# Sign bits in the second score product of a bucketed attention, ahead of two dense layers

## What is computed

```python
q_bits = (np.einsum('bhsd,dk->bhsk', q, proj) > 0).astype(np.int64)
k_bits = (np.einsum('bhsd,dk->bhsk', k, proj) > 0).astype(np.int64)
q_bucket = np.sum(q_bits * powers, axis=-1)
k_bucket = np.sum(k_bits * powers, axis=-1)
mask = q_bucket[:, :, :, None] == k_bucket[:, :, None, :]
scores = scale * np.matmul(q, k.transpose(0, 1, 3, 2))
scores = np.where(mask, scores, -1000000000.0)
attn = np.exp(scores - np.max(scores, axis=-1, keepdims=True))
attn = attn / (np.sum(attn, axis=-1, keepdims=True) + 1e-09)
attn_out = np.matmul(attn, v)
```

## Time and profile before

| | us |
|---|---|
| median of three runs | 784.45 |
| the profiled execution | 782.37 |
| its span on the core | 780.6 |
| attention, to the first output matmul of the dense layers | 262.88 |
| from there to the end | 517.7 |
| TensorE busy (98% of the span) | 763.5 |
| DVE busy (52%) | 405.1 |
| ACT busy (44%) | 343.6 |
| POOL busy (37%) | 288.9 |

### The profile page before, as it was taken

The page is one execution under the profiler, slowest core; times in us unless marked ns, Lnnn a source line. Parts: engine busy times, 40 slices in busy tenths (PEclk is TensorE's granted clock), DMA queues, the critical chain, the costliest instruction groups (busy, mean ns, idle before and its releaser), DMA issues.

```text
span 780.6 us, 12163 instructions
## 1 busy us (share of the span) xinstructions
PE 763.5 (98%) x3800; PEld 644.7 (83%) x3800; DVE 405.1 (52%) x688; ACT 343.6 (44%) x657; POOL 288.9 (37%) x230
## 2 busy tenths in 40 slices
PE   7999999999999999999999999999999999999998
PEld 6788888888889888888888888888888888888886
DVE  5888887888898574343333432352323333242333
ACT  7988898888987221232212322132221312222121
POOL 3688878878897493000000366660000000000000
PEclk9999999999999999999999999999999999999999
DMA  6576667666762342000000032310001000010001
GB/s 168 136 148 167 146 141 177 151 127 157 157 120 61 84 136 82 1 0 1 1 0 1 27 100 89 107 55 0 1 1 42 11 0 0 0 54 0 0 0 54
DMA packets 46312, 52.77 MB, mean 68 GB/s; under 512 B 8912, under 2 KB 34768, under 8 KB 46288
## 3 DMA queue, kind: packets, MB, share of 16 engines
q1 hardware_dynamic: 46064, 52.13, 27.0%
q10 hardware_dynamic: 224, 0.33, 0.2%
HBM read 32.73 MB, written 3.19 MB: 46 GB/s over the span
## 4 chain that ended last, share of the span: by engine, by line
PE 75%; DMA 8%; POOL 6%; issue 5%; SPq 3%; DVE 2%; ACT 0%; POOLq 0%; DVEq 0%
PE acc L594 33%; PE h_ps L576 32%; DMA inv_dram<-row_inv 4%; DMA all_inv<-inv_dram 3%; PE pt_ps L542 2%; POOL wa_lo L431 2%; POOL kt L385 2%; PE pv_ps L556 2%; PE pv_ps L557 1%; PE s_ps L528 1%; PE s_ps L529 1%; POOL wa_hi L429 1%; POOL pt_hi L395 1%; DMA w_raw<-w_out_dram 1%; DVE w_raw L837 1%
## 5 line engine op out<-in xcount | busy, mean ns | idle before, releaser
L770 ACT ACTIVATE r_sb<-h_ps 128x512 f32<-128x512 f32 x96 | 57.4, 598 | 368.0 <-PE h_ps L576 368.0
L909 DVE TENSOR_SCALAR g_sb<-e_sb,sb_scale 128x512 f32<-128x512 f32 x48 | 27.9, 582 | 158.2 <-ACT e_sb L773 158.2
L907 DVE SCALAR_TENSOR_TENSOR g_sb<-e_sb,h_ps 128x512 f32<-128x512 f32 x48 | 33.0, 687 | 135.6 <-ACT e_sb L773 135.1
L804 DVE TENSOR_REDUCE row_min<-s_ps 128x1 f32<-128x768 f32 x96 | 91.5, 954 | 10.3 <-PE s_ps L529 9.6
L693 ACT ACTIVATE probs<-s_ps,row_min 128x768 f32<-128x768 f32 x96 | 87.0, 906 | 11.3 <-DVE row_min L804 9.3
L542 PE MATMUL pt_ps<-cst,probs 128*128 128x128 f32 x576 | 80.8, 275 | 0.7 <-DVE pt_lo L811 0.5
L556 PE MATMUL pv_ps<-pt_hi,v_nat 128*128 128x384 f32 x192 | 72.6, 378 | 7.8 <-DVE w_raw L837 7.7
L576 PE MATMUL h_ps<-xt_hi,wa_lo 128*128 (+1 forms) x192 | 74.7, 389 | 0.0
L576 PE MATMUL h_ps<-xt_lo,wa_hi 128*128 (+1 forms) x192 | 74.7, 389 | 0.0
L576 PE MATMUL h_ps<-xt_hi,wa_hi 128*128 (+1 forms) x192 | 74.7, 389 | 0.0
L576 PE MATMUL h_ps<-xt_hi,wb_hi 128*128 (+1 forms) x192 | 74.7, 389 | 0.0
(11 more groups left out here) (93 smaller groups left out, 1598.3 us busy)
## 6 DMA issues: line engine op xcount, KB each, us to landing
qt<-kt SPq DMA_DIRECT2D x45, 192.0 KB, 3.0
w_raw<-w_in_dram SPq DMA_DIRECT2D x32, 256.0 KB, 2.7
w_raw<-w_out_dram SPq DMA_DIRECT2D x32, 256.0 KB, 2.9
all_inv<-inv_dram SPq DMA_DIRECT2D x32, 192.0 KB, 3.7
raw<-qk_dram SPq DMA_DIRECT2D x15, 384.0 KB, 4.3
raw_v<-v_dram SPq DMA_DIRECT2D x16, 192.0 KB, 4.7
out_dram<-o_sb SPq DMA_DIRECT2D x12, 256.0 KB, 2.1
kt<-kt SPq DMA_DIRECT2D x15, 192.0 KB, 3.7
```

Source lines behind the costliest of these rows:

```text
L804: nc.vector.tensor_reduce(row_min[:, k:k + 1], s_ps[k % 2][:, :, 0:HALF], AX.XY, ALU.min).then_inc(min_done, 1)
```

## The change

**Bits in place of buckets.** Each head's six sign matmuls now stand together in the last unit of the head before (SIGN_UNIT). They make 108 rows in prep_ps: for either half of the tokens 12 rows for q and 12 for k, a bit and its opposite. One DVE operation writes them as 0 or 2^31 (for k -2^31) in fp32r (to_bits, write_bits). Four DMAs of 12 x 384 lay them in rows 64 to 75 of qt2 and kt2 (copy_bits), so the second score product, now over 76 rows, adds -2^62 for each bit in which q and k differ. Counts, onehots, penalties and the scaling of q are gone.

**Scores copied.** DVE multiplies the scores by -1/8 under a ceiling of 2^56, writes them to one of three buffers probs in SBUF and takes their minimum in the same operation (keep_scores); the exponential works in place there, and the next scores wait for the copy.

**Inverse.** POOL adds the epsilon (add_eps), and DVE takes the reciprocal in the first unit of the next group. The put writes single numbers to (t p) order, so that the normalise reads all_inv in sequence.

**Lists.** SyncE's pair and POOL's pair are ordered anew. Weights are loaded and split only in pairs 0 and 7, so five slots are loaded and four split when the attention ends (AMID = 4). In the first head the signs are two fp32 matmuls on the raw q and k (first_signs), and ACT, POOL and DVE make its parts; DVE, POOL, ACT and SyncE lists at the start follow that. WARM is 10 for 12.

SyncE's functions and its pair:

```diff
-            def copy_q(head, par):
-
-                hi, lo = kt1[par][low, :].bitcast(F32), kt2[par][low, :].bitcast(F32)
+            def copy_q_hi(head, par):
+
+                hi = kt1[par][low, :].bitcast(F32)
                 sp.wait_ge(qk_hi, head)
                 sp.dma_start(qt1[par][top, :].bitcast(F32), hi).then_inc(q_copied, 16)
                 sp.dma_start(qt2[par][top, :].bitcast(F32), hi).then_inc(q_copied, 16)
+
+            def copy_q_lo(head, par):
                 sp.wait_ge(qk_split, head)
-                sp.dma_start(qt1[par][low, :].bitcast(F32), lo).then_inc(q_copied, 16)
+                sp.dma_start(qt1[par][low, :].bitcast(F32), kt2[par][low, :].bitcast(F32)).then_inc(q_copied, 16)
...
-                sp.wait_ge(z_done, head + 1)
+                sp.wait_ge(z_done, head)
...
+
+            def copy_bits(head, par):
+
+                sp.wait_ge(bits_done, head)
+                for n in range(2):
+                    cols = slice(n * HALF, (n + 1) * HALF)
+                    for at, dst in ((n * HALF_ROWS, qt2), (n * HALF_ROWS + K_ROWS, kt2)):
+                        sp.dma_start(dst[par][bit_rows, cols].bitcast(F32),
+                                     bits[at:at + BIT_PAIR, :].bitcast(F32)).then_inc(bits_copied, 16)
...
-                sp.dma_start(inv_d[par].rearrange("(p t) -> p t", p=P),
-                             row_inv[:, (g % GROUPS) * HT:(g % GROUPS + 1) * HT]).then_inc(inv_out[par], 16)
+                sp.dma_start(inv_d[par].rearrange("(t p o) -> p t o", p=P, o=1),
+                             row_inv[:, (g % GROUPS) * HT:(g % GROUPS + 1) * HT].unsqueeze(2),
+                             allow_slow_non_contiguous=True).then_inc(inv_out[par], 16)
...
-            def pair(i, prev=True, nxt=True, after=True):
+            def pair(i, prev=True, nxt=True, after=True, weights=()):
                 copy_k(2 * i + 1, 1)
+                copy_bits(2 * i + 1, 1)
                 if prev:
+                    get_inv(i, -1)
                     move_second(i - 1, 0)
-                    get_inv(i, -1)
                 put_inv(i, 0)
                 load_v(2 * i + 1)
+                if weights:
+                    load_w(0, weights[0], 0, weights[0])
+                get_inv(i, 0)
                 if nxt:
-                    copy_q(2 * i + 2, 0)
+                    copy_q_hi(2 * i + 2, 0)
                 if prev:
                     move_second(i - 1, 1)
-                get_inv(i, 0)
+                if nxt:
+                    copy_q_lo(2 * i + 2, 0)
                 if after:
                     load_qk(2 * i + 4, 0)
-                if nxt:
-                    load_w(0, i + 1, 0, i + 1)
                 put_inv(i, 1)
                 if nxt:
                     copy_k(2 * i + 2, 0)
+                    copy_bits(2 * i + 2, 0)
+                get_inv(i, 1)
                 move_first(i, 0)
-                get_inv(i, 1)
                 put_inv(i, 2)
+                get_inv(i, 2)
                 if nxt:
                     load_v(2 * i + 2)
-                    copy_q(2 * i + 3, 1)
+                    copy_q_hi(2 * i + 3, 1)
                 move_first(i, 1)
-                get_inv(i, 2)
+                if nxt:
+                    copy_q_lo(2 * i + 3, 1)
                 if after:
                     load_qk(2 * i + 5, 1)
+                if weights:
+                    load_w(0, weights[1], 0, weights[1])
                 put_inv(i, 3)
```

POOL:

```diff
+            def add_eps(i, g):
+
+                c = slice(g * HT, (g + 1) * HT)
+                pool.wait_ge(exp_done, HT * (GROUPS * i + g) + HT)
+                pool.nop(nofuse=True)
+                nc.gpsimd.tensor_scalar(row_inv[:, c], row_sum[:, c], EPS, 1.0, ALU.add, ALU.mult).then_inc(sum_done, 1)
...
-            def pair(i, prev=True, nxt=True):
+            def pair(i, prev=True, nxt=True, weights=()):
                 split_third(i, 0)
-                split_w(at(wa_hi, i), at(wa_lo, i), i, 0, i + 1)
+                add_eps(i, 0)
+                if weights:
+                    split_w(at(wa_hi, weights[0]), at(wa_lo, weights[0]), weights[0], 0, weights[0] + 1)
+                if prev:
+                    split_x(i - 1, 0)
                 if nxt:
                     split_qk(2 * i + 2, 0)
+                add_eps(i, 1)
                 split_third(i, 1)
                 if prev:
-                    split_x(i - 1, 0)
+                    split_x(i - 1, 1)
                 split_third(i, 2)
+                add_eps(i, 2)
                 split_v(2 * i + 1, 1)
-                if prev:
-                    split_x(i - 1, 1)
+                if weights:
+                    split_w(at(wa_hi, weights[1]), at(wa_lo, weights[1]), weights[1], 0, weights[1] + 1)
                 if nxt:
                     split_qk(2 * i + 3, 1)
+                add_eps(i, 3)
                 split_third(i, 3)
                 if nxt:
                     split_v(2 * i + 2, 0)
...
-            pair(0, prev=False)
+            pair(0, prev=False, weights=(0, 1))
...
-            pair(PAIRS - 1, nxt=False)
+            pair(PAIRS - 1, nxt=False, weights=(2, 3))
```

TensorE:

```diff
+            def first_signs():
+
+                pe.wait_ge(planes_built, 4)
+                pe.wait_ge(k0_in, 16)
+                pe.wait_ge(q0_in, 16)
+                for n in range(2):
+                    last = mm(s_ps[1][0:K_ROWS + BIT_PAIR, n, 0:HALF], planes[:, 0:K_ROWS + BIT_PAIR],
+                              raw[0][:, n * HALF:(n + 1) * HALF], start=True, stop=True)
+                last.then_inc(z0_done, 1)
...
+                wait(pe, bits_done, head - 1)
                 dst = prep_ps[0:SIGN_ROWS, 0:HALF]
-                mm(dst, planes_hi[:, plane], kt1[par][:, cols], start=n == 0, stop=False)
-                mm(dst, planes_lo[:, plane], kt1[par][:, cols], start=False, stop=False)
-                if first:
-                    pe.wait_ge(lo0_done, n + 1)
-                last = mm(dst, planes_hi[:, plane], kt2[par][:, cols], start=False, stop=n == 1)
-                if n == 1:
-                    last.then_inc(z_done, 1)
...
-                mm(bank[:, 0:HALF], code[rows, :], bits[rows, :], start=True, stop=True).then_inc(counts_done, 1)
...
-                wait(pe, exp_done, u - 1)
+                wait(pe, scores_kept, u - 1)
                 q1 = qt1[par][:, t * P:(t + 1) * P]
-                q2 = qt2[par][:, t * P:(t + 1) * P]
+                q2 = qt2[par][score_rows, t * P:(t + 1) * P]
...
                     mm(s_ps[buf][:, n, 0:HALF], q1, kt1[par][:, cols], start=True, stop=False)
-                    last = mm(s_ps[buf][:, n, 0:HALF], q2, kt2[par][:, cols], start=False, stop=True)
+                    last = mm(s_ps[buf][:, n, 0:HALF], q2, kt2[par][score_rows, cols], start=False, stop=True)
...
-                        buckets_out(2 * head + 2)
                         pe.wait_ge(q_copied, 48 * head)
                         pe.wait_ge(k_copied, 16 * head)
+                        pe.wait_ge(bits_copied, 64 * head)
...
                 transpose_probs(i, u, k, 0)
                 transpose_probs(i, u, k, 1)
-                if follows and t == CODE_A:
-                    counts(head, 0)
-                if follows and t == CODE_B:
-                    buckets_out(2 * head + 1)
...
-                if follows and t == SIGN_B:
-                    if first and k == 0:
-                        signs(head, par, 0)
-                    signs(head, par, 1)
-                if more and t == SIGN_A:
-                    buckets_out(2 * head + 2)
-                    signs(head + 1, 1 - par, 0)
-
+                if first and k == 0:
+                    signs(head, par)
+                if more and t == SIGN_UNIT:
+                    signs(head + 1, 1 - par)
```

ACT and DVE:

```diff
-                act.wait_ge(min_done, u + 1)
-                wait(act, pt_done, 2 * u - 2)
-                nc.scalar.activation(probs[k % 2][:].rearrange("p (n c) -> p n c", n=2), s_ps[k % 2][:, :, 0:HALF],
-                                     ACT.Exp, bias=row_min[:, k:k + 1], scale=-1.0,
-                                     accum_out=row_sum[:, k, 0:1]).then_inc(exp_done, 1)
+                act.wait_ge(scores_kept, u + 1)
+                scores = probs[k % SRING]
+                nc.scalar.activation(scores[:], scores[:], ACT.Exp, bias=row_min[:, k:k + 1], scale=-1.0,
+                                     accum_out=row_sum[:, k:k + 1]).then_inc(exp_done, 1)
...
+            def to_bits(dst, z, rows):
+                return ts(dst, z, planes_in_sb[rows, C_THR:C_THR + 1], planes_in_sb[rows, C_AMP:C_AMP + 1], ALU.is_gt,
+                          ALU.mult)
+
...
             def write_bits(head):
...
+                rows = slice(0, SIGN_ROWS)
+                dve.wait_ge(z_done, head)
+                wait(dve, bits_copied, 64 * head - 64)
+                to_bits(bits[:], prep_ps[rows, 0:HALF], rows).then_inc(bits_done, 1)
+
+            def keep_scores(u, k):
+
```

(24 more changed lines are left out.)

318 lines of the change are left out of this document (146 added, 172 removed).

## The result

The changed kernel takes 978.56 us (median of four runs, 975.99 to 981.5), the kernel before 783.97 beside it: 1.248 times the time, 95% interval 1.244 to 1.252. The forecast was 775.0 with a range of 760 to 784. The profiled run has a span of 975.6 us.

A forecast was written before the change was run, and what follows sets the result against it. TensorE was taken to bound the attention, SyncE's queue second. Head -1.7, pair 0 -1.8, six pairs -10.6, last pair -0.4 and tail +5.0 made -9.5 from 784.45: 775.0 us, range 760 to 784.

The forecast's parts named there:

- The put: Inverse row sums to DRAM: 384 pieces of 4 bytes land in 4.3 us, bounds 3.8 and 6.2, for 3.8 before.
- The rival with the slow put: Inverse's way to DRAM: a put longer by x costs 13x; at 100 ns a piece 789.3 us; chance 0.15.
- TensorE bounds the attention, so work taken off it comes off the time: Attention: TensorE is the bound, SyncE's queue second; count matmuls, 0.45 us each, leave the path, 1.8 us per pair.
- the largest term, 10.6 us less in the six pairs: Six middle pairs: 28.7 us each against 30.46, 1.76 x 6 = 10.6 us less.
- SyncE's list in a middle pair: Middle pair: bits ready at 2.5 us, four bit DMAs to 4.7, then get and moves of x, landed at 9.05.
- New stall 1.4 us: Middle pair, unit 5: next head's signs wait 1.4 us for POOL's split of q and k, bounds 0.7 and 1.8.
- Head and pair 0: Start: 1.7 us less from shorter prologue and earlier score bank release, bounds 0 and 3; pair 0 loses its counts, 1.8.
- The tail: Before the first output matmul: last put waits for a weight split and lands behind 512 KB; 5.0 us more, bounds 1 and 7.
- DVE's copy of scores at 1.0 us: DVE in the attention: the copy with minimum takes 1.0 us, bounds 0.95 and 1.15, hidden under TensorE, booked at nothing.
- Signs with 108 columns and scores with 76 rows: TensorE in the attention: 108 columns for 44 and 76 rows for 128 cost nothing, matmuls staying 0.17 us apart.
- The weights not yet split: Dense layers: four slots ready for eight, splits hidden; uncovered up to 3.6 us per slot.
- the fourth rival: Tail: TensorE idles nearly 5 us, its clock halves; 2.7 us more per twelve matmuls, 777.7 us; 3 in 10 within the forecast.

The follow-up runs named there:

- e1: Changed kernel with the put back to 128 pieces of 12 bytes and the normalise reading with a stride; 819.44 us, 1.045 of the kernel before.
- e14: Changed kernel with the 12-byte put, SyncE's pair in the old order and two bit DMAs per head for four; 789.22 us, 1.0065 of the kernel before.
- e17: e15 with the sum and the reciprocal back on DVE in the last unit of a group; 788.32 us, 1.0073 of the kernel before.
- e15: e14 with the last pair's second weight split behind POOL's last sum and third, its load behind SyncE's moves; 786.5 us, 1.0031 of the kernel before.
- e2: Kernel before with only the put in 384 pieces of 4 bytes and the normalise reading in sequence; 916.59 us, 1.170 of the kernel before.

## Why the prediction was wrong

**The put: priced by the wrong time.** "I take 3.8 + 0.5 = 4.3 us, with bounds of 3.8 and 6.2" is the step that failed first: it measured 9.7. The 32 ns per piece of the earlier trace rows are the time that packets occupy a DMA engine; what SyncE waits for is the landing, and the row that held it, 3.8 us for 128 pieces, was not read as a price that depends on how the pieces lie. The trace of before has small neighbouring pieces in this one form only, and the bound was set by what a queue carries, not by what a write waits for. The rival with the slow put had the right side and the right place, at a chance of 0.15 and a price of 789 us. Its formula also fell: 13 x (9.7 - 4.3) = 70 us more would have been 845. It counted two delays per pair. In the new order all four puts of a pair follow each other in one list, and e1 to after is 19.5 us per pair (53.8 - 34.3), near to four times 6.1, less what is hidden.

**TensorE bounds the attention, so work taken off it comes off the time: wrong.** This is the deeper error, and the largest term, 10.6 us less in the six pairs, rests on it. They took 182.75 us with the counts, and 182.34 in e14, without counts and with the put of before. The stretches of the six pairs, before and in e14 (us, busy time and count of PE, PEld, DVE, ACT, POOL, then clock, DMA share, GB/s):

```profile
42.53:225.28 182.75, 175.51 (x1106) 155.34 (x1104) 153.64 (x277) 161.28 (x337) 151.47 (x132) 1.00 0.68 150
47.97:230.31 182.34, 168.36 (x1082) 159.94 (x1081) 145.74 (x312) 137.69 (x301) 135.28 (x142) 0.99 0.62 137
```

TensorE is busy for 7.1 us less and idle for 6.7 us more; its waits for normalised outputs in the pairs grew from 6.5 to 13.6 us. So the work that was saved came back as waiting. I read TensorE's busy time as the bound and booked nothing for what it would wait for next. What sets these waits in e14 is not settled. SyncE waits there for its own DMAs only 5.3 us, less than the 16.0 before, so it is not the list as in the kernel after. On the way to the normalised output POOL's sum and a reciprocal one unit later now stand ahead of the put and the get; e17 took both back, and 14.4 us of these waits stayed. No run takes the counts alone out of the kernel before.

**SyncE's list in a middle pair: wrong.** My walk had the bits ready at 2.5 and let four bit DMAs follow at once. The copy of k stands ahead of them, and it waits for copies of q that themselves now stand behind a get and its put. In e1 the first score matmul of a pair goes at 151.98 and the first bit DMA at 157.62: 5.6 us after it, not 2.5. "New stall 1.4 us" at the signs, behind POOL's split, did not come: TensorE was late by then. In its place there were 4.2 us of waits per pair in unit 4 (1.7 for the bits and 2.5 for the normalised output; 13.5 and 17.8 us in 8 and 7 waits in all) and half a clock behind them.

**Head and pair 0: wrong in sign.** The first scores start at 11.24 us (before: 10.34), the third ones at 14.16 for 13.35, still behind DVE for 1.36 us. Up to there 0.8 us were lost where I took 1.7 off. Pair 0 was to save 1.8 more. In e14 start and pair 0 take 47.97 us for 42.53, 5.4 more, which is the largest part of what e14 loses; TensorE's longest wait there, 3.2 us, is for an output of a group whose put stands behind 512 KB of weights. In e17 the stage takes 41.95, so the later reciprocal has a part in it.

**The tail: half right.** The last put behind a weight load that waits for a split is worth 2.7 us (e15 against e14, with the reservation made there) where I took 5.0, within the bounds of 1 and 7. In the kernel after the wait before the first output matmul is 6.3 us, with the slow put in it.

**Right:** DVE's copy of scores at 1.0 us. It takes 0.955 us with a row of its own of 0.083 for the accumulator, on DVE for the kernel after:

```profile
L813 DVE TENSOR_SCALAR_CACHE_REDUCE probs<-s_ps 128x768 f32<-128x768 f32 x96 | 91.6, 955 | 49.8 <-PE s_ps L562 48.6
...
L813 DVE DVE_READ_ACCUMULATOR probs<-s_ps 128x1 f32 x96 | 8.0, 83 | 0.0
```

The Trainium skill, "VectorE: DVE Perf Modes", section "Two Vector instructions with no wait between them", has it as two instructions; the trace agrees, at 83 ns and not ACT's 201. Together that is 1.04 us. TensorE hardly waited for DVE's splits, until e17 gave DVE more to do. Signs with 108 columns and scores with 76 rows cost nothing, at 0.17 us apart. The weights not yet split stayed hidden: the dense layers took 520.4 us for 517.7, and TensorE waited there for no split. The 2.7 us more are the fourth rival, the clock, at its price of 2.7 us for twelve matmuls: the first twelve, behind the wait of 6.3 us, start 0.43 us apart, not 0.23.

**The clock** was a rival for the tail alone. It came in every pair: the mean granted clock of each of e1's six middle pairs is 0.90, and in one of them, behind two waits, TensorE was granted 0.50 (1.2 GHz) for 4.3 us, and 1.00 again after it (us, busy time and count of five engines, clock):

```profile
160.00:166.20 6.20, 2.01 (x13) 1.43 (x11) 0.92 (x4) 2.86 (x6) 0.66 (x1) 0.84 0.52 85
166.20:170.50 4.30, 4.26 (x15) 4.20 (x16) 2.83 (x7) 1.57 (x4) 3.62 (x4) 0.50 0.72 151
```

Before that TensorE had been idle for two thirds of 6.2 us. 4.3 us at half clock are 2.15 us lost in this pair, an estimate from its row. Over the six pairs TensorE is busy for 179.5 us in e1 and for 168.4 in e14, 1.8 us a pair. So a stall that opens costs more than its own length.

## What to carry to other kernels

Price a small DMA write by its landing, not by the time its packets take, and measure it before it goes on a path that four waits per loop depend on; of the forms tried here, 4-byte pieces side by side in DRAM were the worst. Where one engine issues DMAs in order, read what it waits for: here it was other engines for most of the time before, and its own DMAs for 182 of 186 us of waits when its list held everything up; a get right behind its put then stops all else. Before work taken off the busiest engine is booked as gain, ask what that engine would wait for next: here 7.1 us of saved work became 6.7 us of waiting.

## What the runs showed of the hardware

- 384 pieces of 4 bytes side by side in DRAM land in 9.7 us, 64 bytes apart in 2.6, 512 bytes apart in 2.7; 128 pieces of 12 bytes side by side in 3.6. In the put looked at, the DMA engines are idle for 5.6 of 7.7 us.
- Other DMAs land later as well while such puts are under way: the copies of q took 5.9 us in the kernel after, 4.7 in e1; in the kernel before they took 3.0, and 7.9 with the put alone changed (e2). The Trainium skill, "DMA: Bandwidth & Descriptors", section "Queues, rings and completion order", has a semaphore's write wait for every earlier write of its DMA engine, which would give this; the runs don't show it apart from fuller queues.
- Score matmuls with 64 rows in turn with 128 start 0.37 us apart, with 76 rows 0.17. With 64 rows the load of the weights (0.18 to 0.19 us) starts together with its matmul's record, with 76 rows 0.17 us ahead of it. Why is not shown.
- The accumulator output of a DVE tensor_scalar costs 0.083 us.
- Behind waits TensorE was granted 0.50 of its clock (1.2 GHz) for 4.3 us in e1, and twelve matmuls of 512 columns then start 0.43 us apart for 0.23 in the kernel after.
